# Two mixtures of experts in one stream: 24 slots of 208 to 240 tokens, the second mixture in two passes

## The reference

```python
def _moe_ref(x, w_skip, w_gate, w1, w2):
    do_compute = x @ w_skip > 0
    out = x.copy()
    xc = x[do_compute]
    logits = xc @ w_gate
    e_idx = np.argmax(logits, axis=1)
    probs = softmax(logits); gate_w = probs[np.arange(len(xc)), e_idx]
    for e in range(8):
        mask = e_idx == e
        h = np.maximum(xc[mask] @ w1[e], 0.0)          # 384 -> 1024
        y[mask] = gate_w[mask, None] * (h @ w2[e])     # 1024 -> 384
    out[do_compute] = xc + y
    return out

def _moe2_ref(x, expert_emb, tau, w1, w2):
    logits = (x / (norm(x) + 1e-6)) @ (expert_emb / (norm(expert_emb) + 1e-6)).T / tau
    e_idx = np.argmax(logits, axis=1)
    probs = softmax(logits); gate_w = probs[np.arange(N), e_idx]
    for e in range(8):
        mask = e_idx == e
        out[mask] = gate_w[mask, None] * (np.maximum(x[mask] @ w1[e], 0.0) @ w2[e])
    return out
```

## Time and profile before

| what | value |
|---|---|
| median of 3 runs | 937.52 us (937.01 to 937.58) |
| profiled execution, own time | 936.06 us |
| its span | 934.1 us |
| mean granted TensorE clock | 0.868 |
| PE busy | 706.2 us (76%) |
| DVE, ACT, POOL busy | 603.4, 467.9, 183.9 us |

### The profile page before, as it was taken

One profiled execution on the slowest core, in us unless ns is written; L12 is line 12 of the kernel. 1 busy time (PEld: TensorE's weight loads), 2 busy tenths in 40 slices (PEclk: granted clock), 3 DMA queues, 4 the chain that ended last, 5 costly groups with the idle time before them and its releaser, 6 DMA issues. The chain is left out here.

```text
span 934.1 us, 15941 instructions
## 1 busy us (share of the span) xinstructions
PE 706.2 (76%) x5543; PEld 637.1 (68%) x5543; DVE 603.4 (65%) x1225; ACT 467.9 (50%) x705; POOL 183.9 (20%) x201
## 2 busy tenths in 40 slices
PE   3344341099998999932999999903899999999994
PEld 2233221088888888832999999902799999999994
DVE  3599999667889998867555566536255445535530
ACT  6688986555776777622455555510234323423410
POOL 4000000211221211102044343312111320331211
PEclk9765665577999999975999999955899999999998
DMA  6121220462223223254465445314044254334100
GB/s 165 38 76 44 71 64 0 51 101 77 85 89 97 90 79 101 76 88 153 149 210 193 166 159 174 136 18 160 27 160 148 67 171 151 104 134 146 38 26 25
DMA packets 66024, 95.87 MB, mean 103 GB/s; under 512 B 12630, under 2 KB 51648, under 8 KB 65792
## 3 DMA queue, kind: packets, MB, share of 16 engines
q1 hardware_dynamic: 59584, 81.26, 29.0%
q0 software_dynamic: 6400, 14.12, 4.6%
HBM read 82.71 MB, written 13.55 MB: 103 GB/s over the span
## 5 line engine op out<-in xcount | busy, mean ns | idle before, releaser
L1359 DVE SCALAR_TENSOR_TENSOR hT_lo<-banks,hT_hi 128x448 fp32r<-128x448 f32 (+1 forms) x96 | 62.1, 647 | 148.1 <-ACT hT_hi L1274 124.9
L1274 ACT ACTIVATE hT_hi<-banks 128x448 fp32r<-128x448 f32 (+1 forms) x96 | 54.0, 562 | 203.5 <-PE banks L1227 184.3
L1227 PE MATMUL banks<-xT_hi,w_hi 128*128 128x256 f32 (+1 forms) x384 | 127.7, 333 | 7.5 <-issue 5.7
L1244 PE MATMUL banks<-w_hi,hT_hi 128*128 128x384 f32 (+1 forms) x384 | 132.8, 346 | 0.0
L1244 PE MATMUL banks<-w_hi,hT_lo 128*128 128x384 f32 (+1 forms) x384 | 129.4, 337 | 0.0
L1244 PE MATMUL banks<-w_lo,hT_hi 128*128 128x384 f32 (+1 forms) x384 | 129.2, 336 | 0.0
L1227 PE MATMUL banks<-xT_hi,w_lo 128*128 128x256 f32 (+1 forms) x384 | 126.0, 328 | 0.0
L1227 PE MATMUL banks<-xT_lo,w_hi 128*128 128x256 f32 (+1 forms) x384 | 126.0, 328 | 0.0
L639 PE MATMUL banks<-sq,ident 128*128 128x288 f32 x128 | 59.4, 644 | 86.0 <-ACT sq L573 86.0
L639 PEld LDWEIGHTS banks<-sq,ident 128*128 128x128 f32 x128 | 38.9, 315 | 105.3 <-ACT sq L573 85.5
L1227 PEld LDWEIGHTS banks<-xT_hi,w_hi 128*128 128x128 f32 x384 | 73.6, 192 | 11.8 <-issue 8.1
(11 more groups left out here) (194 smaller groups left out, 1441.2 us busy)
## 6 DMA issues: line engine op xcount, KB each, us to landing
raw<-w1a SPq DMA_DIRECT2D x8, 1536.0 KB, 6.3
raw<-w2a SPq DMA_DIRECT2D x8, 1536.0 KB
raw<-w1b SPq DMA_DIRECT2D x8, 1536.0 KB, 6.4
raw<-w2b SPq DMA_DIRECT2D x8, 1536.0 KB, 7.5
ring<-a SPq DMA_DIRECT2D x9, 864.0 KB, 4.8
qk<-q SPq DMA_DIRECT2D x48, 96.0 KB, 2.2
qk<-k SPq DMA_DIRECT2D x48, 96.0 KB, 2.2
vt<-v SPq DMA_DIRECT2D x24, 192.0 KB, 2.4
```

The source lines that it names most:

```text
L1227: last = pe.matmul(pU[g % TURNS][:, n * CAP:(n + 1) * CAP], w1p[m][:, b, c, f * P:(f + 1) * P], xT[s][:, c, :], start=(c == 0 and (s, m) = ...
L1244: last = pe.matmul(pY[s][0:sizes[s], 0:DM], hT[r][:, f, s * P:s * P + sizes[s]], w2p[m][:, b, f, :], start=(f == 0 and (r, m) == PASSES[0] ...
L1274: act.activation(hT[0][:, g * FB:(g + 1) * FB, :].rearrange("p c t -> p (c t)"), pU[g % TURNS], ACT.Relu).then_inc(h_hi, 1)
L1359: dve.scalar_tensor_tensor(hT[1][:, part, :].rearrange("p c t -> p (c t)"), pU[g % TURNS], 0.0, hT[0][:, part, :].rearrange("p c t -> p (c ...
```

## The change

The lists and both mixtures become one block, `mixtures`, in which every engine walks through one `stream` of slots. The stream has three phases (`Phase`): mixture 1 with slots of 224 tokens; mixture 2 for the skipped tokens, 208; mixture 2 for the computed tokens and for those skipped tokens that had no room in their expert's slot, 240. Each phase has one slot for each expert. Phases 0 and 2 have, besides, a loop for overflow slots, whose tables are filled by 24 indirect stores (`store_overflow`); with the counts above no overflow slot is needed, but the tables are cleared, filled and read. The list work is cut into pieces which stand inside the slots. Skipped tokens have their scores for mixture 2 already from the attention, so the lists of phase 1 need nothing from mixture 1.

In the second product w2 becomes stationary and the hidden units move, so it has 8 x 3 x 3 = 72 matmuls of 224, 208 or 240 columns, and its result has features on partitions. ACT copies it (`keep_y`), PE turns it back (`turn_y`) in the next slot, and DVE multiplies by the gate (`finish`). Scores of mixture 2 are stored in the same row as x (`xbuf` has 384 + 9 columns), in one indirect store.

Core of the diff; a line of "..." marks what is left out:

```diff
-    xbuf = nc.dram_tensor("xbuf", [NT, DM], F32, kind="Internal").ap()
-    scores = nc.dram_tensor("scores", [NT, E + 1], F32, kind="Internal").ap()
+    xbuf = nc.dram_tensor("xbuf", [NT, DM + E + 1], F32, kind="Internal").ap()
...
-                for par in range(2):
-                    sp.wait_ge(x_stored[par], 16 * (UNITS // 2 + 1 + par))
...
+                for old in retired:
+                    pool.sem_clear(old)
...
+                dve.tensor_reduce(logits[:, 1:UNITS - 1, 0:NR], shares[:, 1:UNITS - 1].rearrange("p u g e -> p u e g"),
+                                  AX_X, ALU.add)
                 mask(UNITS - 1, 1)
                 dve.wait_ge(logit_copied, UNITS + 2)
-                dve.tensor_reduce(logits[:, 1:, 0:NR], shares[:, 1:].rearrange("p u g e -> p u e g"), AX_X, ALU.add)
+                dve.tensor_reduce(logits[:, UNITS - 1:, 0:NR], shares[:, UNITS - 1:].rearrange("p u g e -> p u e g"),
+                                  AX_X, ALU.add)
...
+        phases = [Phase(nc, ctx, 0, 224, NT, E, (w1a, w2a), xbuf, True, True),
+                  Phase(nc, ctx, 1, 208, NT, E, (w1b, w2b), out, False, False),
+                  Phase(nc, ctx, 2, 240, NT, E, (w1b, w2b), out, False, True)]
...
+        def _(sp):                                       # SP
+            sp.dma_start(xbuf[:, DM:]..., logits[:, 1:, E + 1:]).then_inc(table_stored, 16)
+            weights.load(sp, Slot(phases[0], 0, 0, 0, 0), None, 0)
+            sp.wait_ge(blank_set, 1)
+            for ph in phases:
+                if ph.dynamic:
+                    sp.dma_start(ph.table.rearrange("(c p) e -> p c e", p=P), blank[:, 0:ph.OVER * SUB, :]
+                                 ).then_inc(ph.table_cleared, 16)
+            def body(slot, before, older, nxt):
+                weights.load(sp, nxt, slot, e)
+                if ph.n == 1 and slot.at == 0:
+                    for s in range(SUB):
+                        sp.wait_ge(before.ph.scattered[s], before.j * 16 + 16)
+                    sp.dma_start(routing[:, :, :], xbuf[:, DM:]...).then_inc(routing_loaded, 16)
+                if ph.dynamic and slot.at == 3:
+                    sp.wait_ge(ph.overflow_stored, 16 * UNITS)
+                    sp.dma_start(loaded..., ph.table...).then_inc(ph.overflow_loaded, 16)
...
+            def body(slot, before, older, nxt):          # POOL
+                if before is not None:
+                    pool.wait_ge(before.ph.y_ready, before.j * SUB + SUB)
+                pool.wait_ge(ph.x_turned, slot.j * SUB + SUB)
+                gather(nxt)
+                scatter(before)
+                if (ph.n, slot.at) == (0, 1): store_overflow(ph, range(0, 12))
+                if (ph.n, slot.at) == (0, 2): store_overflow(ph, range(12, UNITS))
+                if (ph.n, slot.at) == (1, 7): store_overflow(phases[2], range(0, 6))
+                if (ph.n, slot.at) == (2, 0): store_overflow(ph, range(6, 15))
+                if (ph.n, slot.at) == (2, 1): store_overflow(ph, range(15, UNITS))
...
+            def body(slot, before, older, nxt):          # PE
+                ph, N, b = slot.ph, slot.ph.CAP, slot.b
+                pe.wait_ge(ph.lo1_ready, slot.j * 2 + 2)
+                pe.wait_ge(ph.x_lo, slot.j * SUB + SUB)
+                for g in range(NG):
+                    if g >= TURNS:
+                        pe.wait_ge(ph.h_lo, slot.j * NG + (g - TURNS + 1))
+                    ... 18 matmuls of N columns, w1 stationary
+                    if before is not None and g < SUB:
+                        turn_y(before, older, g)
+                pe.wait_ge(ph.lo2_ready, slot.j * 2 + 2)
+                for f in range(FC):
+                    if f % 2 == 0:
+                        pe.wait_ge(ph.h_lo, slot.j * NG + (f // 2 + 1))
+                    for c in range(KC):
+                        for s, m in PASSES:
+                            last = pe.matmul(turned(c)[:, 0:N], w2p[m][:, b, f, c * P:(c + 1) * P], hT[s][:, f, 0:N], ...)
+                    if f in (2, 4) and nxt is not None:
+                        turn_x(nxt, f // 2 - 1)
+                if (ph.n, slot.at) == (0, 0): list_tokens(ph, 2, 5, GATE, ph.gated)
+                if (ph.n, slot.at) in ((0, 2), (1, 3)): rank_tokens(phases[ph.n + 1])
+                if (ph.n, slot.at) in ((0, "close0"), (1, 6)): list_tokens(phases[ph.n + 1], 0, 5, ENTRY, ...)
...
+            def body(slot, before, older, nxt):          # DVE
+                hidden(slot, 0); finish(before, older, 0)
+                if at == (0, 0): weights.lo_part2(dve, slot, 0)
+                weights.lo_part1(dve, nxt, 0)
+                hidden(slot, 1)
+                if at == (0, 0): weights.lo_part2(dve, slot, 1)
+                finish(before, older, 1)
+                ... overflow at (0, 1), tabulate at (0, 2), index and gates at (0, "close1") and (1, 7)
+                hidden(slot, 2); weights.lo_part1(dve, nxt, 1); hidden(slot, 3)
+                ... share and weigh at (0, 0); choose at (0, 2); place, remain and share at (0, 3);
+                ... weigh and spots at (0, "close0"); choose (1, 3), place (1, 4), share and weigh (1, 5),
+                ... spots (1, 6), overflow (1, 7), tabulate (2, 1)
+                weights.lo_part2(dve, nxt, 0); split_x(nxt, 0)
+                weights.lo_part2(dve, nxt, 1); split_x(nxt, 1)
+                if ph.dynamic and slot.at == 3: adopt(ph)
```

More of the change, by code:

```diff
@@ L419, in build @@
         consts = (token_hi, down, iota, iota_b, part_no, resets, after, ones)
[L420 to L426, removed]
+        mixtures(nc, xbuf, out, x_stored, [16 * (UNITS // 2 + 1 + par) for par in range(2)], logits, consts, ident,
+                 wr2, banks, w1a, w2a, w1b, w2b)
     return nc
@@ L825, with hi_part1 @@
-PAD = 4096
-def assign(nc, which, logits, consts, banks, lists, weights, scores, rows):
-    token_hi, down, iota, iota_b, part_no, resets, after, ones = consts
-    E, UNITS = down.shape[1], token_hi.shape[1]
-    CAP, SUB, SLOTS, COLS = lists.CAP, lists.SUB, lists.SLOTS, lists.COLS
-    MOST = -(-UNITS * P // CAP)
+    def hi_part1(self, act, slot, half):
+        act.wait_ge(slot.ph.loaded1, slot.j * 16 + 16)
+        act.copy(self.part(self.hi1[:, slot.b], half), self.part(self.raw1[:, :, :], half)
+                 ).then_inc(slot.ph.hi1_ready, 1)
@@ L857, in assign @@
[L857 to L858 removed]
+        starts = sbuf("starts", EU)
         begin = sbuf("begin", [P, UNITS])
[L860 to L866 removed]
@@ L943, in _ @@
+            for half in range(2):
+                weights.hi_part1(act, head, half)
+            for half in range(2):
+                weights.hi_part2(act, head, half)
+            for s in range(SUB):
+                split_x(head, s)
+            tail, second = stream(act, phases, E, body)
+            keep_y(tail)
         @block.vector
@@ new lines, in remain, with spots @@
+            def remain(ph):
+                done(dve.tensor_scalar(left[:, :], logits[:, 1:, E], 0.0, None, ALU.is_le))
+                done(dve.scalar_tensor_tensor(left[:, :], rank[:, :], float(ph.CAP), left[:, :],
+                                              ALU.is_lt, ALU.mult))
+                done(dve.tensor_scalar(left[:, :], left[:, :], -1.0, 1.0, ALU.mult, ALU.add))
+            def spots(ph):
+                for u in range(UNITS):
+                    last = dve.tensor_scalar(spot[:, u, :], iota_b[:, :], inside[:, u:u + 1], None, ALU.is_equal)
+                    if u % CHUNK == CHUNK - 1:
+                        last.then_inc(ph.spotted, 1)
@@ new lines, in weigh, with gates @@
+            def weigh(ph):
+                for n in range(3):
+                    last = dve.tensor_tensor(entry[:, :, 2 + n, :], reach[:, :, :], per_token(values[:, n], LOW),
+                                             ALU.mult)
+                last.then_inc(ph.weighed, 1)
+            def gates(ph):
+                dve.wait_ge(ph.gated if ph.n == 0 else ph.listed, 1)
+                done(dve.tensor_reduce(ph.gate[:, 0:LOW], pL[:, GATE:GATE + 3 * LOW].rearrange("p (a s) -> p s a", a=3),
+                                       AX_X, ALU.add))
@@ L1420 @@
+            head = Slot(phases[0], 0, 0, 0, 0)
+            choose(head.ph)
+            place(head.ph)
+            spots(head.ph)
+            index(head.ph)
+            for half in range(2):
+                weights.lo_part1(dve, head, half)
+            for s in range(SUB):
+                split_x(head, s)
+            tail, second = stream(dve, phases, E, body)
+            for s in range(SUB):
+                finish(tail, second, s)
 def kernel(**inputs):
```

1167 lines of the change are left out of this document (601 added, 566 removed).

## The result

The changed kernel takes 1029.18 us (median of 4 runs, 1026.37 to 1034.59) where the kernel before takes 937.55 in the same rounds: the ratio is 1.0986, 95% interval 1.0939 to 1.1032. It is slower by 92 us; 928.4 was predicted, with 948 as the upper end. The profiled execution took 1026.37 us, its span is 1024.6.

What follows compares the result with a forecast made beforehand. Both mixtures were taken as bound by PE, with the distance between matmul starts as unit. 427.7 to the first matmul, 0.5, 485.9 of stream and 10.9 of tail gave 925.0 us of span, 928.4 measured; range 920 to 937, with rivals 900 to 948.

Steps and rivals of the forecast that it cites:

- 29.6, 1.5 and 14.5: Stream: stalls and PE work from list pieces inside slots 29.6 us, late gather in (1,1) 1.5, first slot 14.5.
- the prediction's own sign: Stalls in the stream: wrong if starts follow the columns, or if POOL's gathers or SP's w1 release most stalls.
- the stall behind `share` and `weigh`: First slot: DVE still owes this list work after its second half of `lo_part2`, stalling PE 4.8 us.
- the 6.3 for `lo2_ready`: First slot: PE waits 6.3 us (1.3 to 11), as DVE's `lo_part2` queues behind the split of a late w1.
- The third rival: First slot and stream: cleared tables hold the queue 14 us, clock stays low after each stall; about 940 us, chance 0.1.
- the first two rivals: Products: columns set the pace, 103 ns and less, about 903 us, chance 0.15; pace 118 ns, about 944 us, chance 0.18.
- the fifth: Products: fp32r with under 256 columns falls to the plain fp32 rate, about 1858 us, chance 0.04.
- the floor of the weight load: Products: below 256 columns the weight load is the limit, 112 ns between matmul starts for 208, 224 and 240 columns.
- E - 1.5: Slots with list work: E us of it on DVE ahead of the splits stalls PE for E minus 1.5 us of slack.
- the fourth rival: Slots with list work: its stalls hide, -29.6 + 4 us, about 903 us, chance 0.08.

Runs made afterwards that it cites:

- experiment 1: Changed kernel with the load of w1 issued only when the token rows of the next slot have landed: 987.98 us.
- experiment 2: Changed kernel loading only 32 columns of w1 and of w2 after the first slot, same casts and products on old data: 963.08 us.
- experiment 4: Changed kernel whose gathers wait for the y of the slot before only behind scored slots: 978.8 us.
- experiment 9: Changed kernel, overflow kept: w1 behind gathers, earlier gathers, list work behind casts, w2 moving in mixture 2, later clearing, stores over three slots: 933.61 us.
- Experiment 3: Changed kernel without overflow machinery: no tables, clearing, indirect stores, loop or register reads, fixed slot counts: 977.63 us.
- experiment 6: Changed kernel without overflow machinery, with w1 held behind gathers, gathers not waiting for `finish`, and a third row buffer: 923.43 us.
- version 8: Changed kernel without overflow, w1 behind gathers, earlier gathers, third row buffer, list work behind casts, w2 moving in mixture 2's second product: 885.57 us.

## Why the prediction was wrong

By the terms of the sum, in us of the profiled span (a wait is a gap of 0.45 us or more between matmuls of the stream; the predicted 37 are 29.6, 1.5 and 14.5 without 1.8 of clock and 6.8 of PE's own list work):

| term | predicted | measured |
|---|---|---|
| first matmul | 428.2 | 444.3 |
| products at full clock | 387.1 | 379 |
| turns, scores, PE's part of the lists | 55 | 56 |
| waits of PE in the stream | 37 | 100 |
| slower clock after waits | 7 | 29 |
| stream in all | 485.9 | 564.3 |
| tail | 10.9 | 16.0 |

**The step that failed** is in the part on POOL: "The next gather lands 14 us in; PE wants it at 13. So 48 stores cost only about 1 us at each of two slots". Two of its inputs were wrong. The gather was given some 2.3 us to land: the prediction does not print the figure, but the expectation of experiment 1 does, and POOL's end 10.7 us in (7.1 + 7.2 + 15.5, less a slot of 19.1), 1.1 for the copied index and 2.3 make its 14. It is the median of the kernel before, over the only four gathers of that trace whose landing is known: three with no load beside them, 2.0 to 2.5 us, and one beside 1.7 MB of weights, 6.0. The prediction had what it takes to see it. Its slot loads 3 MB at 177 GB/s, so 1.5 MB of w1 are on their way in every slot, and nothing in it kept them off the gather. And the trace of the kernel before showed the collision in mixture 1. There a gather is issued at 507.80, 2.6 us behind a load of w2, and this is all that the engines moved from 507.8 to 510.8:

```profile
q1 hardware_dynamic: 764, 1.17, 104.4%
```

The gather's queue starts only then; that kernel had the slack for it. `finish` did end where predicted, 7.05 us in (955.85 in the chain of slot (2,5)). The gather was issued 1.5 us later, 8.6 us in, and PE wanted the rows at 11.7; with 2.3 us for landing 0.8 would have been in hand (2 in phases 0 and 1, where the turn comes at 13 to 14). The 7.9 that it took make a stall of 4.7. Waits over 2 us stand in 18 of the 23 slots that turn rows for a next one. In 14 of them the landing of rows ends the wait; in (0,0), (0,6), (1,4) and (1,6) it is DVE's `xT_lo`, as predicted. By the prediction's own sign (wrong if another queue releases most stalls) the mechanism failed. Experiments 1, 2 and 4 show it from three sides (41, 66 and 50 us; they touch the same waits and don't add up). The largest misses of this kind are (2,4), 8.9 us where none was predicted, and (1,1), 1.6 and 8.3 where 1.5 was. The second input was the stores. Most come every 1.29 us, but the instructions of three of the twelve took 1.5 to 2.2 us in place of 0.98; the twelve took 17.8 us (487.9 to 505.7) and in experiment 9 19.4, in place of 15.5, behind 8.3 us of POOL's own work in place of 7.2. Why single ones take longer is open: in experiment 2, with hardly a load running, they do too. They ended 15.0 us into the next slot, where 10 was predicted. Experiment 3 puts the whole machinery, with the head's part, at 51.6 us.

**The first matmul.** Of the 16.1 us, 3.0 come before the lists: they start at 408.9, not 405.9 (406.3 to 409.9 in the versions here, whose attention is the same). 1.2 more lie in the lists (index at 422.7, 13.8 us after). The rest is the first gather:

```profile
411.76 14.62 SPq L992 DMA_DIRECT2D over_table<-mix_blank  x2
427.00 9.41 SPq L762 DMA_DIRECT2D raw<-w1a  x1
```

```profile
424.32 2.06 POOL mix_rows L1040
426.38 0.31 issue
426.69 15.62 DMA mix_rows<-xbuf,to_gather
442.31 0.04 issue
442.36 0.92 PE banks L1137 x3
```

The clearing of the tables, issued at 411.8 (first fence, SP's timeline), took 24.2 to 24.6 us to land, not 9 in all, and the gather issued at 426.69 (second fence, the chain) landed at 442.3 behind it and behind the w1 of the next slot. The prediction asked what the clearing does to the load of w1 and put its cost into the first slot; it fell on the gather, one step earlier. From the start of the lists to the first matmul it is 35.4 us here, 31.4 with w1 held back (experiment 1), 25.4 without the tables (3) and 21.7 without either (6); 22.3 was predicted. Slot (0,0) itself took 27.6 us, 31.5 predicted: the stall behind `share` and `weigh` came (5.4 us, 4.8 predicted), the 6.3 for `lo2_ready` shrank to 0.5. The third rival (tables hold the queue 14 us, clock stays low) was of the right kind, with a far too small price: +12 for what is some 10 at the head (experiment 3) and 22 of clock.

**The clock** was put at 1.8 us for the first slot and 5 for all others. It was paid in 16 second products, 215.3 us for all 24 in place of 189, and in the first product of (0,0).

**The tail** is 5.1 us longer. Last product to last store 4.3 us in place of 3.2; last store to the end 11.7 in place of 7.7. The cause of these 4 us was not looked for; it is 11.7 or 11.8 in every version with the overflow and 10.8 in every one without, so it belongs to the program.

**What held.** 112 ns for 208 to 240 columns, so the first two rivals and the fifth fall, as the floor of the weight load said; the products cost what they cost before, 17.35 to 17.75 us for a plain slot and 18.7 for a scored one (17.75 and 19.1 predicted); and the list stalls by "E - 1.5" in five of seven slots, to within 0.3 us. In the two with `place` they are 2.6 and 1.8 longer, 6.8 in (0,3) and 3.5 in (1,4), since `place` takes 4.9 us there and not 3.2. All seven are 23.3 us of waits in experiment 6, where DVE's part of the 29.6 had 19.2 for them; so the fourth rival falls too. With the collisions removed (experiment 6) the kernel takes 923.4 us against the 928.4 predicted. Part of this agreement is luck, as that kernel also has no overflow work, and its longer list stalls and slow clock stand against that.

So the change's own gains (53.6 us of lists as a stretch, 16.5 at the head) were there to be had: version 8, with six more edits, is 52 us below the kernel before, but for lists that fit their slots. For any routing only 4 us are left (experiment 9): the overflow's stores on POOL's queue and the late `adopt` are the parts of the loss that are known, and the best order with the overflow kept stays open.

## What to carry to other kernels

A transfer's landing time is no constant: give it the value that it has when the largest load of the same stretch is in flight, and look which of both is issued first. When slots get shorter, every wait whose slack was never measured becomes a candidate; add up the slack of each slot at its tightest point (here 0.8 to 2 us for the gather) before adding up the gains. And what a stream of small indirect transfers costs is the delay of the first urgent one queued behind it, not its own duration.

## What the runs showed of the hardware

- A gather of 128 rows, issued 1.5 us ahead of a load of 1.5 MB, had no packet moved for 5.4 us and landed after 7.9. With that load held back the median gather lands after 3.7 (experiment 1), with hardly any load after 3.3 (experiment 2). In the kernel before, one issued while 1.2 MB of weights were still coming had no packet moved for the first 3.0 us.
- Writing 6656 pieces of 8 bytes, in two transfers, took 24.6 and 24.2 us to land; the two gathers issued 12.6 and 14.9 us after the first landed after 12.2 and 15.6 us.
- The POOL instruction of a gather took 0.96 us at best, 1.86 in the median of 32, and 2.46 at most; with the gathers out of that stretch (experiment 4) it is 1.07 in the median, and 1.13 in the same place of the slot with hardly any load (experiment 2).
- The last indirect store of the kernel before was issued 7.7 us ahead of the end, that of the changed kernel 11.7, though its rows had moved after 2.4.
- A wait of 4.8 us left the clock at 0.98 while it lasted, and it stood at 0.50 for the 3.2 us behind it.
